# Sending token names to slots in a top-1 mixture-of-experts kernel: one-hot rows of 64 with a 6-bit and 3-bit split of the slot number, in place of rows of 128

## What is computed

```python
# x: [3072, 384] from the attention stage; E = 8 experts, cap = 3072 // 8 = 384
logits = x @ w_gate
order = np.argsort(-logits.flatten())
for idx in order:                       # highest logit first
    tok, e = idx // E, idx % E
    if assigned[tok] >= 0 or counts[e] >= cap:
        continue
    assigned[tok] = e
    counts[e] += 1
for e in range(E):
    out[assigned == e] = np.maximum(x[assigned == e] @ w1[e], 0.0) @ w2[e]
h = out @ w_in
result = (h * np.clip(h + 3.0, 0.0, 6.0) / 6.0) @ w_out
```

## Time and profile before

| | before |
|---|---|
| median of the runs | 870.23 us (866.92 to 873.95) |
| the profiled execution's own time | 869.4 us |
| its span | 867.7 us |
| mean granted clock of TensorE | 0.968 |
| PE busy | 799.1 us (92%) |
| DVE busy | 597.6 us (69%) |
| ACT busy | 350.7 us (40%) |
| POOL busy | 269.0 us (31%) |

### The profile page before, as it was taken

How to read it: one execution, slowest core, us unless ns; L and a number is a source line. 1 busy time by engine, 2 the same in 40 slices (tenths; PEclk the granted TensorE clock), 3 DMA queues, 4 the chain that set the end, 5 groups by cost and what they waited for, 6 DMA issues and landing times.

```text
span 867.7 us, 17171 instructions
## 1 busy us (share of the span) xinstructions
PE 799.1 (92%) x6196; PEld 764.2 (88%) x6196; DVE 597.6 (69%) x1130; ACT 350.7 (40%) x759; POOL 269.0 (31%) x299
## 2 busy tenths in 40 slices
PE   5999999316988999999999999999999999999996
PEld 5999998205988999999999999999999999999995
DVE  7999999687786568756865676677568656762210
ACT  3777776102433423433352335234423432343332
POOL 4443433001356303430251144124303420341233
PEclk9999999657999999999999999999999999999998
DMA  7566662013303201210130022012201310130000
GB/s 289 198 219 215 213 214 105 25 48 125 122 25 122 79 0 48 100 51 0 48 124 27 0 82 91 27 48 76 76 0 48 100 51 0 58 114 28 1 1 27
DMA packets 22405, 70.00 MB, mean 81 GB/s; under 512 B 3040, under 2 KB 9312, under 8 KB 22368
## 3 DMA queue, kind: packets, MB, share of 16 engines
q1 hardware_dynamic: 19296, 60.06, 19.9%
q0 software_dynamic: 3072, 9.44, 3.3%
HBM read 60.05 MB, written 9.44 MB: 80 GB/s over the span
## 4 chain that ended last, share of the span: by engine, by line
issue 38%; PE 20%; POOL 16%; DVE 5%; POOLq 1%; ACT 1%; DMA 0%; DVEq 0%; ACTq 0%
PE ps L1025 19%; POOL act_lo L673 11%; POOL out L687 2%; POOL rows L648 2%; DVE at_q L787 1%; POOL this_ids L668 1%; POOL w_out_lo L661 0%; DVE at_q L876 0%; DMA rows<-x_rows,gather_ids 0%; POOLq L639 0%; DVE place L847 0%; PE ps L1016 0%; PE ps L985 0%; POOLq L672 0%; ACT act_hi L742 0%
## 5 line engine op out<-in xcount | busy, mean ns | idle before, releaser
L673 POOL TENSOR_TENSOR act_lo<-gate,act_hi 128x384 fp32r<-128x384 f32 x128 | 133.1, 1042 | 373.4 <-ACT act_hi L742 373.2
L737 ACT ACTIVATE gate<-ps,three 128x384 f32<-128x384 f32 x128 | 74.5, 582 | 231.6 <-PE ps L1025 213.6
L1025 PE MATMUL ps<-yT_hi,w_in_hi 128*128 128x384 f32 x384 | 132.8, 346 | 4.3 <-DVE gate L944 2.6
L1025 PE MATMUL ps<-w_out_hi,act_hi 128*128 128x384 f32 x384 | 130.8, 341 | 5.2 <-POOL act_lo L673 5.2
L1025 PE MATMUL ps<-yT_hi,w_in_lo 128*128 128x384 f32 x384 | 130.2, 339 | 0.0
L1025 PE MATMUL ps<-yT_lo,w_in_hi 128*128 128x384 f32 x384 | 129.7, 338 | 0.0
L1025 PE MATMUL ps<-w_out_hi,act_lo 128*128 128x384 f32 x384 | 129.1, 336 | 0.0
L1025 PE MATMUL ps<-w_out_lo,act_hi 128*128 128x384 f32 x384 | 129.1, 336 | 0.0
L944 DVE SCALAR_TENSOR_TENSOR gate<-gate,ps 128x384 f32<-128x384 f32 x128 | 70.8, 553 | 84.6 <-ACT gate L737 81.2
L723 ACT ACTIVATE act_hi<-ps 128x384 fp32r<-128x384 f32 x64 | 31.5, 492 | 138.6 <-PE ps L1025 136.0
L927 DVE SCALAR_TENSOR_TENSOR act_lo<-ps,act_hi 128x384 fp32r<-128x384 f32 x64 | 35.6, 556 | 75.3 <-ACT act_hi L723 75.3
(11 more groups left out here) (177 smaller groups left out, 1597.3 us busy)
## 6 DMA issues: line engine op xcount, KB each, us to landing
raw<-in_w SPq DMA_DIRECT2D x48, 512.0 KB
attn_wrk<-in_wrk SPq DMA_DIRECT2D x24, 770.5 KB, 4.6
attn_v<-in_v SPq DMA_DIRECT2D x24, 192.0 KB, 4.4
x_rows<-attn_x SPq DMA_DIRECT2D x24, 192.0 KB, 1.9
raw<-in_w_in SPq DMA_DIRECT2D x6, 512.0 KB
raw<-in_w_out SPq DMA_DIRECT2D x6, 512.0 KB
rows<-x_rows,gather_ids POOLq DMA_INDIRECT x24
out<-rows,scatter_ids POOLq DMA_INDIRECT x24
```

Of the source, the lines that this page charges most:

```text
L673: pool.tensor_tensor(act[1][:, (H1 + g) % 3, :], gate[:, g % 2, :], act[0][:, (H1 + g) % 3, :].bitcast(F32), ALU.subtract).then_inc(g_lo, 1)
L737: act_.activation(gate[:, g % 2, :], mid[g % 2], ACT.Relu, bias=three[:, 0:1]).then_inc(gate_relu, 1)
L1025: last = pe.matmul(out_, w, d, start=start and n == 0, stop=stop and n == len(passes) - 1)
```

## The change

The slot is split into 6 low bits and 3 high bits. The one-hot rows are 64 wide in place of 128, and `names` has six groups (`GROUPS`) in place of three thirds. PE then holds the one-hot rows of two tiles at once, as the counting does, and moves both tiles' 24 columns of `names`: 12 matmuls in place of 24. Of the result only two blocks mean something, the even tiles' (partitions 0 to 63, columns 0 to 11) and the odd tiles' (partitions 64 to 127, columns 12 to 23). DVE copies the odd block, adds the even block, and then writes each of the two id tensors in two halves of 64 partitions.

```diff
             def name(e):
-                over_t = [128, TILES, ET]
+                over_t = [128, TILES, GROUPS]
-                link(dve.tensor_scalar(slot_q[:, :], slot_i[:, :], 127, None, ALU.bitwise_and))
-                link(dve.tensor_scalar(slot_t[:, :], slot_i[:, :], 7, None, ALU.logical_shift_right))
+                link(dve.tensor_scalar(slot_q[:, :], slot_i[:, :], J - 1, None, ALU.bitwise_and))
+                link(dve.tensor_scalar(slot_t[:, :], slot_i[:, :], 6, None, ALU.logical_shift_right))
...
             def name_q(e, half):
                 tiles = halves[half]
-                shape = [128, TILES // 2, 128]
-                dve.tensor_tensor(at_q[:, tiles, :], to_127[:, :].unsqueeze(1).to_broadcast(shape),
+                shape = [128, TILES // 2, J]
+                dve.tensor_tensor(at_q[:, tiles, :], to_63[:, :].unsqueeze(1).to_broadcast(shape),
...
             def take_ids(e):
                 dve.wait_ge(named, e + 2)
-                link(dve.tensor_copy(ids_f[:, :], ids_ps[:, ET:2 * ET]))
-                dve.scalar_tensor_tensor(gather_ids[:, :], ids_ps[:, 0:ET], float(PT), ids_f[:, :], ALU.mult, ALU.add)
-                dve.scalar_tensor_tensor(new_ids[:, :], ids_ps[:, 0:ET], float(PT), ids_f[:, :],
-                                         ALU.mult, ALU.add).then_inc(ids_ready, 1)
+                link(dve.tensor_copy(odd_ids[:, :], ids_ps[J:2 * J, 2 * GROUPS:4 * GROUPS]))
+                link(dve.tensor_tensor(all_ids[:, :, :, :].rearrange("q c t h -> q (c t h)"), ids_ps[0:J, 0:2 * GROUPS],
+                                       odd_ids[:, :], ALU.add))
+                for ids in (gather_ids, new_ids):
+                    for h in range(2):
+                        last = dve.scalar_tensor_tensor(ids[h * J:h * J + J, :], all_ids[:, 0, :, h], float(PT),
+                                                        all_ids[:, 1, :, h], ALU.mult, ALU.add)
+                last.then_inc(ids_ready, 1)
...
             def send_names(e):
-                for t in range(TILES):
+                for t in range(0, TILES, 2):
                     if t % (TILES // 2) == 0:
                         pe.wait_ge(names_ready, 2 * e + 3 + t // (TILES // 2))
-                    last = pe.matmul(ids_ps, at_q[:, t, :], names[:, t, :, :].rearrange("p c t -> p (c t)"),
-                                     start=(t == 0), stop=(t == TILES - 1))
+                    last = pe.matmul(ids_ps, at_q[:, t:t + 2, :].rearrange("p t q -> p (t q)"),
+                                     names[:, t:t + 2, :, :].rearrange("p t c k -> p (t c k)"),
+                                     start=(t == 0), stop=(t == TILES - 2))
                 last.then_inc(named, 1)
```

More of the change, by code:

```diff
@@ L434 @@
 ET = CAP // PT
+GROUPS = CAP // J
 LAG = 2
@@ L461, in __init__ @@
         self.fill, self.limit = sb("fill", [128, E]), sb("limit", [128, E])
-        self.to_127, self.tile_no = sb("to_127", [128, 128], BF16), sb("tile_no", [128, TILES])
-        self.part_no, self.third_no = sb("part_no", [128, 1]), sb("third_no", [128, ET])
+        self.to_63, self.tile_no = sb("to_63", [128, J], BF16), sb("tile_no", [128, TILES])
+        self.part_no, self.group_no = sb("part_no", [128, 1]), sb("group_no", [128, GROUPS])
         self.open_logits, self.choice = sb("open_logits", [128, TILES, E]), sb("choice", [128, TILES, E], BF16)
@@ L485, in set @@
         pool.iota(self.limit[:, :], [[CAP, E]], base=BASE + CAP, channel_multiplier=0, **iota)
-        pool.iota(self.to_127[:, :], [[1, 128]], base=0, channel_multiplier=0, **iota)
+        pool.iota(self.to_63[:, :], [[1, J]], base=0, channel_multiplier=0, **iota)
         pool.iota(self.tile_no[:, :], [[1, CHUNKS], [CHUNKS, B]], base=0, channel_multiplier=0, **iota)
-        pool.iota(self.third_no[:, :], [[1, ET]], base=0, channel_multiplier=0, **iota)
+        pool.iota(self.group_no[:, :], [[1, GROUPS]], base=0, channel_multiplier=0, **iota)
         pool.iota(self.part_no[:, :], [[0, 1]], base=0, channel_multiplier=1, **iota)
@@ L540, in experts @@
         next_ids, this_ids, done_ids = (sb(n + "_ids", [PT, ET]) for n in ("next", "this", "done"))
+        new_ids = sb("new_ids", [PT, ET])
         TE, ECT = [128, TILES, E], [128, E, 2, TILES]
@@ L546, in experts @@
         rank, one_to_J, not_run, fill, limit = tables.rank, tables.one_to_J, tables.not_run, tables.fill, tables.limit
-        to_127, tile_no, part_no, from_p, ones = tables.to_127, tables.tile_no, tables.part_no, tables.from_p, tables.ones
+        to_63, tile_no, part_no, from_p, ones = tables.to_63, tables.tile_no, tables.part_no, tables.from_p, tables.ones
         restart, shares, slot, waiting = tables.restart, tables.shares, tables.slot, tables.waiting
@@ L557, in experts @@
         cuts = sb("cuts", [128, J])
-        at_q = sb("at_q", [128, TILES, 128], BF16)
-        above = at_q[:, 0:TILES // 2, :].rearrange("p t (h j) -> p (t h) j", h=2)
+        at_q = sb("at_q", [128, TILES, J], BF16)
+        above = at_q
         full_of, full = sb("full_of", [J, E], BF16), tables.full
@@ L566, in experts @@
         q_f, t_f = sb("q_f", [128, TILES]), sb("t_f", [128, TILES])
-        at_t = sb("at_t", [128, TILES, ET])
-        names = sb("names", [128, TILES, 2, ET], BF16)
-        ids_f, new_ids = sb("ids_f", [128, ET]), sb("new_ids", [128, ET])
+        at_t = sb("at_t", [128, TILES, GROUPS])
+        names = sb("names", [128, TILES, 2, GROUPS], BF16)
+        odd_ids, all_ids = sb("odd_ids", [J, 2 * GROUPS]), sb("all_ids", [J, 2, ET, 2])
         ps = ctx.enter_context(nc.psum_tensor("ps", [128, 8, 512], F32))
@@ L578, in experts @@
         within, totals = (ps[:, 2 + i, 0:2 * E * TILES] for i in range(2))
-        ids_ps = ps[:, 4, 0:2 * ET]
+        ids_ps = ps[:, 4, 0:4 * GROUPS]
         moved = sem("moved")
@@ L860, in name @@
             def name(e):
-                over_t = [128, TILES, ET]
+                over_t = [128, TILES, GROUPS]
                 link(dve.tensor_scalar(slot_i[:, :], slot[:, :], pick_base[:, 0:1], None, ALU.subtract))
-                link(dve.tensor_scalar(slot_q[:, :], slot_i[:, :], 127, None, ALU.bitwise_and))
-                link(dve.tensor_scalar(slot_t[:, :], slot_i[:, :], 7, None, ALU.logical_shift_right))
+                link(dve.tensor_scalar(slot_q[:, :], slot_i[:, :], J - 1, None, ALU.bitwise_and))
+                link(dve.tensor_scalar(slot_t[:, :], slot_i[:, :], 6, None, ALU.logical_shift_right))
                 link(dve.tensor_copy(q_f[:, :], slot_q[:, :]))
                 link(dve.tensor_copy(t_f[:, :], slot_t[:, :]))
-                link(dve.tensor_tensor(at_t[:, :, :], tables.third_no[:, :].unsqueeze(1).to_broadcast(over_t),
+                link(dve.tensor_tensor(at_t[:, :, :], tables.group_no[:, :].unsqueeze(1).to_broadcast(over_t),
                                        t_f[:, :].unsqueeze(2).to_broadcast(over_t), ALU.is_equal))
```

## The result

| | before | after |
|---|---|---|
| median of 22 runs each | 870.18 us (866.69 to 874.13) | 868.35 us (864.72 to 870.25) |
| the profiled execution's own time | 869.4 us | 869.7 us |
| its span | 867.7 us | 868.0 us |
| PE busy | 799.1 us | 798.8 us |
| DVE busy | 597.6 us | 596.5 us |

The ratio is 0.9975, with a 95% interval of 0.9963 to 0.9987: 2.2 us less, between 1.1 and 3.2. By the two medians it is 1.8 us. The time lies inside the range (861.5 to 869.5), but the prediction said 865.5, 4.7 us under the median of before. So the direction was right and the size was not. The one profiled execution is even slower than the one of before, so its span says nothing by itself; it has to be cut into stretches.

What follows compares the result with a forecast made beforehand. In a settled phase PE's own instructions were taken to be the time, with DVE's steps bounding the opening search and a late act_lo phase 0. Savings of 1.8 + 1.0 + 1.4 = 4.2 us led to 865.5 us, range 861.5 to 869.5.

Steps and rivals of the forecast that it cites:

- Term 1: Phases 1 to 6: twelve names matmuls less in each, 0.62 to 0.32 us, saving 1.8 us in all.
- Term 2: Opening search on DVE: name +0.22, name_q -1.60, take_ids +0.35 us, together -1.0 us.
- Term 3: Phase 0: shorter name_q lets POOL's last low part of w_out end earlier, so PE restarts 1.4 us earlier.
- about 1.5 us idle are left: Phase 0, before PE's restart: the idle time of 2.63 us was to shrink to about 1.5 us.
- The sum: Whole kernel: 1.8 + 1.0 + 1.4 = 4.2 us saved, with no term for the clock.
- a rival with 0.08: Phase 0: a clock drop to 1.2 GHz falls where nothing covers it, costing 1.7 us, 866.9 us; chance 0.08.
- none came behind the longer idle stretch: Phase 0, kernel before: no clock drop followed the longer idle stretch before 273.87; said within the clock rival.
- The base: Whole kernel: 4.2 us taken from the profiled execution's 869.4 gave 865.2; 865.5 was predicted, the median being 870.23.

Runs made afterwards that it cites:

- halves_order: Changed kernel with take_ids' four last results reordered, both id tensors for partitions 0 to 63, then both for 64 to 127: 867.39 us, ratio 0.9968.
- before_b: The kernel before, unchanged, run once more for its trace alone; no time or ratio is given.
- before_c: The kernel before, unchanged, another run for its trace alone; no time or ratio is given.
- after_c: The changed kernel, unchanged, run for its trace alone; no time or ratio is given.
- phases_new: New form in the seven searches of the phases, old form in the opening search: 867.67 us, ratio 0.9967 to the kernel before.
- before_d: The kernel before, unchanged, one more run for its trace alone; no time or ratio is given.
- open_new: New form in the opening search alone, old form in the phases' seven searches: median 869.29 us, ratio 0.9991 to the kernel before.
- before_early: Kernel before, with SP issuing the expert's first load as soon as its own buffer is free: 868.45 us, ratio 0.9976.

## Why the prediction was right in its parts and wrong in its size

- **Term 1** held. It is 0.32 us for twelve matmuls, phases of 80.8 us in place of 81.07, and 1.7 to 1.8 us against 1.8. The rule of the Trainium skill that was weighed there ("LDWEIGHTS (loading the stationary operand)") would have given 1.3 us for each search; the trace gives 0.30.
- **Term 2** failed in the step on `take_ids`: +0.35 us were worked out and +0.64 measured. The 0.08 us between unlinked instructions was taken from two that write the same partitions; the new four alternate between halves and are 0.17 apart, and the neighbours do not overlap with them either (the copy starts 1.25 us after `w_lo` and not 1.13). The write into the other half was the cost that the text took as nothing. With `name` at +0.17 in place of +0.22 the term is -0.7, not -1.0.
- **Term 3** held nearly in size. POOL's last low part ended 56.9 to 57.0 us behind the first counting in the four traces of before and 55.6 to 55.7 in the five of after, 1.3 us less where 1.38 were worked out; at the restart it is 1.2 on average, with pairs of traces from 0.8 to 1.4. But one sentence of it was wrong: "about 1.5 us idle are left". It is 2.57 us, about the same as before. The forecast let PE arrive at the restart at the old time; in the old trace PE had been slowed by the fall of the clock, and without it PE is there earlier and waits as long. `halves_order` bears this out: it has the new form and a fall behind the first idle stretch, and only 1.91 us idle are left.
- **The sum** is where the prediction failed: it put the clock at nothing. The fall behind the restart was written as a rival with 0.08, with nearly the right price (1.7 us, measured 1.55) and with the right reason why it was free before. Its chance was far too low: it was there in 5 of 5 traces. Before, the stretch at 1.2 GHz lay in covered time in 3 of 4 traces. The step that failed is the sentence that none came behind the longer idle stretch: that was one trace, and `before_b` shows it there. Besides, term 3 was taken to move that stretch and leave the clock as it was. By the counts, the change moves the fall into the open in 1 - 0.25 = 0.75 of the runs, 1.2 us. 3.7 less 1.2 is 2.5 us; measured are 2.2 and 2.4, with intervals from 1.1 to 3.7. Those intervals are wide enough that the size alone would not prove the account; the row from the restart to the names does.
- **The base** was mixed: the sum from the profiled execution gave 865.2 and 865.5 was said, while the median lay 0.8 us above that execution. From the median, 4.2 us would have been 866.0.

Why the fall goes to the second stretch in the changed kernel and to the first one in the old can be narrowed from the same traces. The clock rises to 2.4 GHz 0.9 to 2.5 us before the first counting, and the view by stretches places that rise. With 0.50 ahead of it and 1.00 behind it, a granted clock of 0.78 over 206 to 212 us puts it at about 208.6 us (before_c, first line), and 0.89 at 207.3 (after_c, second); stretches of 1 us give it to a few hundredths.

```profile
206.00:212.00 6.00, 6.00 (x39) 5.47 (x38) 3.73 (x6) 3.18 (x6) 0.00 (x0) 0.78 0.39 132
206.00:212.00 6.00, 6.00 (x42) 5.68 (x41) 3.50 (x9) 1.66 (x3) 0.00 (x0) 0.89 0.33 104
```

Counted from that rise, the second idle stretch began 61.6 to 62.3 us later in all seven traces with a fall behind it (the five of after, phases_new and before_b), and 63.0 to 64.0 us later in the five without one (before, before_c, before_d, open_new and halves_order). The first stretch began 45.7 us (before_b) or 47.1 to 47.4 us behind the rise in the five traces with a fall there (before, before_b, before_c, before_early and halves_order), and 46.4 to 47.0 us in the other eight. So what separates the traces is where the idle stretch lies from the rise, and term 3 itself, by bringing PE's restart 1.2 us nearer, carries the second stretch of the changed kernel to where a fall follows. The one trace of the kernel before that has a fall there, before_b, is the one in which the clock rose late, 0.9 us before the first counting and not 1.8 to 2.5. That was read out of the traces afterwards; no run moved one stretch alone, and why these places and not others stays open, so the cause of the move is not shown.

## What to carry to other kernels

An engine that waits for another may hide a slow stretch, and a change that moves the wait can lay the slow stretch open: price a clock fall wherever the engine idles for some microseconds, and look at several traces before giving it a chance. Small instructions on VectorE that alternate between two halves of the partitions were 0.16 to 0.17 us apart here, and 0.08 us apart where two in a row wrote the same half, so write all results of one half before the other. And packing two matmuls into one saves their start-to-start time in the stream, here 26 ns, and not the length that the profile lists for a weight load.

## What the runs showed of the hardware

- TensorE was at 1.2 GHz for about 3 us after 2.45 to 2.83 us without work, in most executions but not in all, and at either of two such stretches 15 to 17 us apart. Whether a fall followed went with where the stretch began behind the last rise of the clock (61.6 to 62.3 us: seven of seven; 63.0 to 64.0 us: none of five). With 38 small matmuls in each stretch neither of two traces has it.
- Two VectorE instructions of 3 elements per partition started 0.08 us apart when they wrote the same 64 partitions and 0.16 to 0.17 us apart when they did not.
- A VectorE instruction with two SBUF inputs and one of POOL did not run at the same time: POOL's low part of 128 x 1024 took 2.39 to 2.40 us alone, 3.11 beside a `name_q` of 768 elements and 3.90 beside one of 1536. The Trainium skill (SBUF — State Buffer, "Who interferes with whom") calls this an exclusive lock; these rows agree, and in all nine traces of the two kernels POOL's took 3.9 and 3.1 us, as it does when the VectorE instruction that had waited goes first.
- POOL's first indirect gather took 1.24 us beside the earlier trace rows's work, 1.36 in the changed kernel and 1.72 when it began 0.3 us earlier; what it waits for was not tested.
